# Gate logits with the weights held still in four 128x32 tiles, the partial products turned back and summed on VectorE

## The reference

```
attention:  per batch (8) and head (8): x 512x64, state 32x64
            xread = softmax(x state^T / 8) state,  sread = softmax(state x^T / 8) x
            rows = [xread, sread] per batch, heads side by side  -> 4608 tokens x 512
moe:        y = leaky_relu(rows @ w_in (512x2048), 0.01) @ w_out (2048x512)
moe2:       logits = y @ w_gate (512x8);  e = argmax(logits)
            gate = softmax(logits)[e],  eom = sigmoid(y @ w_output_gate (512x8))[e]
            out  = gate * eom * (relu(y @ w1[e]) @ w2[e])         8 experts, 1024 hidden
```

## Time and profile before

| what | value |
|---|---|
| time, median of 3 | 1213.87 us (1213.4 to 1214.17) |
| profiled execution, its own time | 1215.19 us |
| its span | 1212.8 us |
| PE busy | 1172.3 us, 97% |
| PEld (weight loads, beside PE) | 972.4 us, 80% |
| DVE busy | 564.4 us, 47% |
| ACT busy | 396.1 us, 33% |
| granted TensorE clock, mean | 0.994 of full |
| gate logits L531 on PE | 272 records, 32.7 us |

### The profile page before, as it was taken

One profiled execution on the slowest core, in us unless ns is written; L12 is line 12 of the kernel. 1 busy time (PEld: TensorE's weight loads), 2 busy tenths in 40 slices (PEclk: granted clock), 3 DMA queues, 4 the chain that ended last, 5 costly groups with the idle time before them and its releaser, 6 DMA issues.

```text
span 1212.8 us, 18414 instructions
## 1 busy us (share of the span) xinstructions
PE 1172.3 (97%) x6802; PEld 972.4 (80%) x6803; DVE 564.4 (47%) x1254; ACT 396.1 (33%) x743; POOL 160.0 (13%) x200
## 2 busy tenths in 40 slices
PE   5999999999999999999999997999999999999995
PEld 3778778778787777787787886898999989889894
DVE  5574373563654744744734436452222225355221
ACT  4343333333423433433333334141111124244111
POOL 1000001010010010010000104222112122233221
PEclk9999999999999999999999999899999999999998
DMA  9211111111120210110000320453111111533111
GB/s 354 98 40 35 36 40 36 35 40 36 40 70 1 73 37 6 69 36 1 35 1 1 112 81 35 122 203 114 35 52 36 51 53 43 191 99 118 51 37 34
DMA packets 37725, 78.44 MB, mean 65 GB/s; under 512 B 9094, under 2 KB 9350, under 8 KB 37639
## 3 DMA queue, kind: packets, MB, share of 16 engines
q1 hardware_dynamic: 28549, 52.92, 12.5%
q0 software_dynamic: 9120, 24.76, 6.5%
HBM read 59.75 MB, written 20.61 MB: 66 GB/s over the span
## 4 chain that ended last, share of the span: by engine, by line
PE 79%; DVE 13%; ACT 5%; issue 1%; DMA 0%; DVEq 0%; ACTq 0%; POOL 0%; SPq 0%; POOLq 0%
PE bank L462 22%; PE bank L464 22%; PE bank L463 22%; PE bank L531 2%; PE bank L513 2%; PE bank L562 2%; DVE gT_lo L1039 2%; PE bank L482 2%; ACT gT_hi L862 2%; DVE g_buf L1035 2%; PE bank L699 1%; PE bank L523 1%; DVE a_buf L1010 1%; DVE a_buf L1000 1%; ACT a2T L815 1%
## 5 line engine op out<-in xcount | busy, mean ns | idle before, releaser
L462 PE MATMUL bank<-wout_lo,gT_hi 128*128 128x512 f32 x544 | 219.1, 403 | 0.0
L464 PE MATMUL bank<-wout_hi,gT_hi 128*128 128x512 f32 x544 | 212.8, 391 | 0.0
L463 PE MATMUL bank<-wout_hi,gT_lo 128*128 128x512 f32 x544 | 211.9, 390 | 0.0
L462 PE MATMUL bank<-xgT_lo,w_hi 128*128 128x256 f32 x512 | 146.6, 286 | 2.7 <-DVE w_lo L1149 1.1
L464 PE MATMUL bank<-xgT_hi,w_hi 128*128 128x256 f32 x512 | 146.1, 285 | 0.0
L463 PE MATMUL bank<-xgT_hi,w_lo 128*128 128x256 f32 x512 | 146.1, 285 | 0.0
L1035 DVE TENSOR_TENSOR g_buf<-g_buf,bank 128x512 f32<-128x512 f32 (+1 forms) x144 | 94.4, 655 | 107.4 <-ACT g_buf L856 107.2
L856 ACT ACTIVATE g_buf<-bank 128x512 f32<-128x512 f32 (+1 forms) x144 | 82.8, 575 | 183.5 <-PE bank L464 157.7
L1039 DVE TENSOR_TENSOR gT_lo<-g_buf,gT_hi 128x512 fp32r<-128x512 f32 (+1 forms) x144 | 95.5, 663 | 91.4 <-ACT gT_hi L862 90.7
L933 ACT ACTIVATE hT_hi<-bank 128x256 fp32r<-128x256 f32 x128 | 48.9, 383 | 240.6 <-PE bank L464 240.6
L862 ACT CAST gT_hi<-g_buf 128x512 fp32r<-128x512 f32 (+1 forms) x144 | 85.9, 596 | 120.8 <-DVE g_buf L1035 120.8
(11 more groups left out here) (184 smaller groups left out, 1732.3 us busy)
## 6 DMA issues: line engine op xcount, KB each, us to landing
raw<-w_dram SPq DMA_DIRECT2D x20, 1024.0 KB, 8.0
rows_dram<-y_buf SPq DMA_DIRECT2D x8, 1032.0 KB, 4.6
XT<-xT_in_dram SPq DMA_DIRECT2D x8, 1024.0 KB, 5.3
X<-x_in_dram SPq DMA_DIRECT2D x8, 1024.0 KB, 5.1
win<-w_in_dram SPq DMA_DIRECT2D x4, 1024.0 KB, 13.5
y_buf<-w_out_dram POOLq DMA_DIRECT2D x6, 512.0 KB, 6.6
stT<-stT_in_dram SPq DMA_DIRECT2D x8, 128.0 KB, 2.2
yT<-w_out_dram POOLq DMA_DIRECT2D x2, 512.0 KB, 7.6
```

Source lines behind the costliest of these rows:

```text
L462: pe.matmul(o, l_hi, r_lo, start=first, stop=False)
L463: pe.matmul(o, l_lo, r_hi, start=False, stop=False)
L464: return pe.matmul(o, l_hi, r_hi, start=False, stop=last)
```

## The change

For routing r, each of the four turned tiles is kept until all are there. The turned rows of tiles 0 and 1 lie in `yT`, those of 2 and 3 in `scT` (free at that time; in layer 8 in a free part of the arena). `logit_parts` then holds a 128x32 piece of the gate weights still (16 real columns, 16 of no use) and lets 256 turned tokens stream by, in column group c for feature piece c: 4 groups, 2 halves of tokens, 8 fp32 multiplications. The four partial products lie under one another in one PSUM bank, 32 partitions each. ACT copies the bank (`keep_parts`), TensorE turns it back in four transposes (`flip_parts`), and DVE adds the four pieces while reading (`add_logits`). Flip 2 moves from f=4 to the end of f=3 and flip 3 from the end of f=4 to its middle. The logits of the state rows stay as they were (`state_logits`).

```diff
+        late_turned = at("late_turned", [P, 2, DM], fp32, offset=arena + 16 * 1024)
+        late_parts = at("late_parts", [P, DM], fp32, offset=arena + 20 * 1024)
+        def turned_pair(r, q):
+            return yT if q == 0 else scT if r < B - 1 else late_turned
+        def parts_of(r):
+            return a2T[:, 0, :] if r < B - 1 else late_parts
 flip_y:
-                    last = pe.transpose(aux[[0, 1, 1, 0][t]][:, P * c:P * c + P], y_buf[:, t, P * c:P * c + P], ident)
+                    last = pe.transpose(aux[t % 2][:, P * c:P * c + P], y_buf[:, t, P * c:P * c + P], ident)
-            def logits(r, q):
-                pe.wait_ge(yT_ready, 4 * r + 2 * q + 2)
-                for t in (0, 1):
-                    for c in range(DC):
-                        last = pe.matmul(aux[q][:, WG_N * t:WG_N * t + WG_N], yT[:, t, P * c:P * c + P], wg[:, WG * c:WG * c + WG_N],
-                                         start=(c == 0), stop=(c == DC - 1))
+            def logit_parts(r):
+                pe.wait_ge(gates_in, 16)
+                pe.wait_ge(yT_ready, 4 * r + 4)
+                for q in range(2):
+                    for c in range(DC):
+                        last = pe.matmul(aux[0][NS * c:NS * c + NS, PAIR * q:PAIR * q + PAIR], wg[:, WG * c:WG * c + NS],
+                                         turned_pair(r, q)[:, :, P * c:P * c + P], start=True, stop=True)
+                last.then_inc(parts_ps, 1)
+            def flip_parts(r):
+                pe.wait_ge(parts_kept, r + 1)
+                for t in range(4):
+                    last = pe.transpose(aux[1][:, P * t:P * t + P], parts_of(r)[:, P * t:P * t + P], ident)
+                last.then_inc(lg_ps, 1)
 beside_up, f == 4:
-                    flip_y(r, 2)
+                    else:
+                        pe.wait_ge(yT_ready, 4 * r + 2)
+                    flip_y(r, 3)
 beside_down:
   f == 3 
-                    logits(r, 0)
+                    else:
+                        pe.wait_ge(yT_ready, 4 * r + 1)
+                    flip_y(r, 2)
   f == 4 
-                    pe.wait_ge(lg_copied, 2 * r + 1)
-                    flip_y(r, 3)
+                    logit_parts(r)
   f == 5 
-                    logits(r, 1)
+                    flip_parts(r)
   f == 6, before make_v(b, 2)
-                        pe.wait_ge(lg_copied, 2 * r + 2)
+                        pe.wait_ge(lg_copied, r + 1)
 ScalarE
+            def keep_parts(r):
+                act.wait_ge(parts_ps, r + 1)
+                act.copy(parts_of(r)[:, :], aux[0][:, :]).then_inc(parts_kept, 1)
 beside_g:
                 if r is not None and f in (1, 2, 4):
-                    keep_yT(r, f // 2)
+                    keep_yT(r, f - 1)
+                elif r is not None and f == 5:
+                    keep_parts(r)
 layer, after g_step:
-                        if f == 4:
-                            keep_yT(r, 3)
+                        if f == 3:
+                            keep_yT(r, 2)
 VectorE, at f == 5 (before: at f == 3 and f == 5, copy_logits)
+            def add_logits(r):
+                dve.wait_ge(lg_ps, r + 1)
+                parts = aux[1][:, :].rearrange("p (t c e) -> p t e c", t=4, c=DC)
+                dve.reduce_sum(logit[:, :, :], parts[:, :, 0:WG, :], AX.X).then_inc(lg_copied, 1)
```

More of the change, by code:

```diff
@@ L188, in build @@
         yT_ps, yT_ready, lg_ps, lg_copied = sem("yT_ps"), sem("yT_ready"), sem("lg_ps"), sem("lg_copied")
+        parts_ps, parts_kept = sem("parts_ps"), sem("parts_kept")
         dif_ready, edif_ready, hot_ready, z_ready, ez_ready = sem("dif_ready"), sem("edif_ready"), sem("hot_ready"), sem("z_ready"), sem("ez_ready")
@@ L522, in flip_y, with state_logits @@
                 for c in range(DC):
-                    last = pe.transpose(aux[[0, 1, 1, 0][t]][:, P * c:P * c + P], y_buf[:, t, P * c:P * c + P], ident)
+                    last = pe.transpose(aux[t % 2][:, P * c:P * c + P], y_buf[:, t, P * c:P * c + P], ident)
                 last.then_inc(yT_ps, 1)
-            def logits(r, q):
+            def logit_parts(r):
                 pe.wait_ge(gates_in, 16)
-                pe.wait_ge(yT_ready, 4 * r + 2 * q + 2)
+                pe.wait_ge(yT_ready, 4 * r + 4)
[9 more added lines that the diff above has]
+                last.then_inc(lg_ps, 1)
+            def state_logits():
+                pe.wait_ge(gates_in, 16)
+                pe.wait_ge(yT_ready, 4 * B + 2)
                 for t in (0, 1):
                     for c in range(DC):
-                        last = pe.matmul(aux[q][:, WG_N * t:WG_N * t + WG_N], yT[:, t, P * c:P * c + P], wg[:, WG * c:WG * c + WG_N],
+                        last = pe.matmul(aux[0][:, WG_N * t:WG_N * t + WG_N], yT[:, t, P * c:P * c + P], wg[:, WG * c:WG * c + WG_N],
                                          start=(c == 0), stop=(c == DC - 1))
@@ L762, in first_step_and_last_routing @@
                 flip_y(B, 1)
-                logits(B, 0)
+                state_logits()
                 pe.wait_ge(xg_lo_done, 2)
@@ L768, in first_step_and_last_routing @@
                         ranks(B, 2, rank_bank=oacc[0])
-                        pe.wait_ge(lg_copied, 2 * B + 1)
+                        pe.wait_ge(lg_copied, B + 1)
                     if f >= 4:
@@ L834, in keep_yT @@
                 act.wait_ge(yT_ps, 4 * r + t + 1)
-                act.copy(yT[:, t % 2, :], aux[[0, 1, 1, 0][t]][:, :]).then_inc(yT_ready, 1)
+                act.copy(turned_pair(r, t // 2)[:, t % 2, :], aux[t % 2][:, :]).then_inc(yT_ready, 1)
+            def keep_parts(r):
+                act.wait_ge(parts_ps, r + 1)
+                act.copy(parts_of(r)[:, :], aux[0][:, :]).then_inc(parts_kept, 1)
             def exp_gates(r, tiles):
@@ L1046, in keep_y, with copy_state_logits @@
                     dve.tensor_copy(y_buf[:, t, 0:DM], acc[t][:, :]).then_inc(y_kept_v, 1)
-            def copy_logits(r, q):
-                dve.wait_ge(lg_ps, 2 * r + q + 1)
-                dve.tensor_copy(logit[:, 2 * q:2 * q + 2, :], aux[q][:, 0:2 * WG_N].rearrange("p (t n) -> p t n", t=2)[:, :, 0:WG]).then_inc(lg_copied, 1)
+            def add_logits(r):
+                dve.wait_ge(lg_ps, r + 1)
+                parts = aux[1][:, :].rearrange("p (t c e) -> p t e c", t=4, c=DC)
+                dve.reduce_sum(logit[:, :, :], parts[:, :, 0:WG, :], AX.X).then_inc(lg_copied, 1)
+            def copy_state_logits():
+                dve.wait_ge(lg_ps, B + 1)
+                dve.tensor_copy(logit[:, 0:2, :], aux[0][:, 0:2 * WG_N].rearrange("p (t n) -> p t n", t=2)[:, :, 0:WG]).then_inc(lg_copied, 1)
             RS = route_steps(4)
@@ L1060, in route @@
                 l1, l2 = logit[:, 0:T, 0:E], logit[:, 0:T, E:2 * E]
-                dve.wait_ge(lg_copied, 2 * r + T // 2)
+                dve.wait_ge(lg_copied, r + 1)
                 step = Steps(dve, route_step, RS * r, 6)
@@ L1159, in layer @@
                     if r is not None:
-                        if f in (3, 5):
-                            copy_logits(r, f // 2 - 1)
+                        if f == 5:
+                            add_logits(r)
                         elif f == 6:
@@ L1310, in _ @@
             rows_lo(0)
-            copy_logits(B, 0)
+            copy_state_logits()
             route(B, 2)
```

## The result

The changed kernel took 1199.53 us (median of 4, 1198.72 to 1200.67) against 1214.02 us for the kernel before: ratio 0.9878, 95% interval 0.9866 to 0.989, 14.5 us less. The forecast was 1199.1 us, with a range of 1197.2 to 1204.5. The profiled execution took 1198.8 us with a span of 1197.0 us, 15.8 us less than the span before.

A forecast was written before the change was run, and what follows sets the result against it. TensorE (PE) alone was taken to set a layer's length. Per routing 3.57 - 1.27 - 0.46 = 1.84 us less, 14.8 us over eight: 1215.2 - 14.8 = 1200.4 us, as a median 1199.1 us, range 1197.2 to 1204.5.

The forecast's parts named there:

- PE sets the length of a layer: Layers: PE busy 83.9 of 84.1 us, so PE work taken out shortens the kernel equally, unless a new wait opens.
- Removed, 3.57 us a routing: Old logits on PE: two calls per routing at 1.79 us each, 3.57 us together, go away.
- `logit_parts`, 1.27 us, four groups at once: New multiplications on PE: four column groups work at once, so a call costs 1.27 us; forecast's chance 0.76.
- The 0.05 us set aside for loads of a tile in use: In `logit_parts`: a tile's second multiplication loads weights only while its first runs; 0.05 us allowed.
- The lower end: Lower bound for a `logit_parts` call: 1.22 us, with nothing for loading the second multiplications' weights.
- Cover of `keep_parts`: ACT's new copy ends before `flip_parts` needs it: 1.3 us cover in layers 1 to 7, 0.17 in layer 8.
- DVE and transfers at nothing: DVE's sum takes 0.4 us, within 39 us of room per layer; no transfer added or moved; no cost.
- First rival, strict order: In `logit_parts`, a record with a busy tile holds back all behind: call 2.29 us, kernel 1207.3 us; chance 0.07.
- the 3.9 us: Length of `make_v` if multiplications start and end strictly in program order: about 9 x 0.43 us.
- Second rival, no concurrency: In `logit_parts`, tiles taking all 128 rows do not overlap: call 3.81 us, kernel 1219.5 us, slower; chance 0.05.
- From execution to median: Whole kernel: median of runs lies 1.3 us below the profiled execution, so 1200.4 us becomes 1199.1 us.

The follow-up runs named there:

- one-group run: Changed kernel with all eight `logit_parts` multiplications in column group 0, summed in PSUM, DVE reading only that piece: 1218.89 us, ratio 1.0037 to the kernel before.
- narrow-stream run: Kernel before, with 32 instead of 96 columns streaming in each multiplication of the old logits: 1213.98 us, ratio 0.9999.
- the run with the other order: Changed kernel with both token halves of a column group directly behind one another, then the next group: 1198.5 us, ratio 0.9871 to the kernel before.
- A second copy: Changed kernel with a second full ACT copy of the bank, into a buffer nobody reads, ahead of `keep_parts`: 1198.88 us, ratio 0.9877 to the kernel before.
- calls of 64: Changed kernel with `read_states` as thirty-two multiplications in one call, four column groups, and one transpose back: 1198.9 us, ratio 0.9858 to the kernel before.
- a kernel that differed in the place of the next waiting transpose: Kernel with `read_states` in two calls of sixteen multiplications (1187.71 us), its transpose moved behind `down(15)`, DVE keeping its result after the y copies: 1184.53 us.

## Why the prediction was right, step by step

- **PE sets the length of a layer.** Held. 3.58 us of old calls less 1.21 and 0.44 is 1.93 us, and the layer is 1.93 us shorter. In the one-group run a call longer by 2.56 us made the layer 2.52 us longer.
- **Removed, 3.57 us a routing.** Held, and the narrow-stream run shows that the columns were not what it paid for.
- **`logit_parts`, 1.27 us, four groups at once.** The mechanism held, as the one-group run shows; the size was 1.21. The 0.05 us set aside for loads of a tile in use was not needed. This and rounding in the flips (0.44, not 0.46) are the 0.09 us a routing by which the sum was short: 14.8 forecast, 8 x 1.93 = 15.4 in the layers.
- **The lower end.** The bound of 1.22 "with nothing for it" was in effect the value. The page "TensorE: Matmul & The Clock Gate" of the Trainium skill, section "Measured speedup vs the span model", gives 2.38 times for three column tiles, from which the prediction made an estimate of 1.09 us of streaming. The trace does not agree for the streaming: 1.21 less the 0.35 for the ends is 0.86 us.
- **Cover of `keep_parts`.** Held in layers 1 to 7. In layer 8 it held partly by luck. The prediction measured its cover against the start of the transposes, 1.58 us after `down`, but their weight loads need the copy and begin at 694.68, 1.34 us after `down` (693.34). A copy ending at 1.41 us, as worked out, would have come 0.07 us late. It ended at 1.24, because it began 0.27 us after the scaling and not 0.43, and 0.1 us of cover was left. A second copy used it up and cost 0.2 us once.
- **DVE and transfers at nothing.** Held: the sum takes 0.425 us where 0.4 was said, and in the stretch after layer 8 PE is busy for 7.41 of 14 us as before.
- **First rival, strict order.** Wrong, but the argument against it was weaker than the prediction put it. In `make_v` no tile is used by two multiplications, so all eight can start in the order of the program and still overlap; rows 5 then do not contradict the rule that the prediction quoted from the Trainium skill, and the 3.9 us that the prediction drew from it holds only if the rule is read for records and not for multiplications. The run with the other order is the proof.
- **Second rival, no concurrency.** Worked out at 1219.5 us; made on purpose it took 1218.9.
- **From execution to median.** The profiled executions differ by 16.4 us in time (15.8 in span), the medians by 14.5: the execution profiled before lay 1.2 us above its median, the one after 0.7 below. So the forecast's closeness (0.4 us) owes something to chance; the layers show an error of 0.6 us over all eight routings.

## What to carry to other kernels

Look for multiplications with few moving columns whose records follow each other 0.11 us apart under 128x128 weights. There cutting columns gives nothing, but holding the narrow operand still in four column groups turned 3.57 us into 1.21 plus 0.44 for turning back. Price it by the cost of entering and leaving (0.35 us a call) and by one group's streaming, and check the way back: a copy and a transpose need cover on their engines, and the cover ends where the weight load starts, not where the multiplication does. Calls of 16 and 32 narrow records ran without gaps here, calls of 64 in three cases of eight; nothing between was tried. A wait for the answer that stood 24 plain multiplications behind the call cost nothing, one that stood 12 behind cost 0.4 to 0.5 us in six layers.

## What the runs showed of the hardware that was not expected

- The four column groups of 128x32 tiles stream beside one another at no cost: 0.86 us for all four, 3.42 us for the same work in one.
- Multiplications for a free column group start ahead of an earlier one whose group is busy: the call costs 1.21 us in one order and 1.23 in the other.
- 64 records of narrow multiplications in a row stalled in five of eight calls, with gaps of 0.16 to 0.5 us (1.1 in two calls) after some 42 records. After two of the five the granted clock fell to 0.50 to 0.60 of full in stretches of 2 us, and plain multiplications stepped at 0.43 us for 3 to 3.5 us. Calls of 32 records did not stall.
- A signal came 3.0 us after the records that gave it had ended, DVE and the queue of the next X load both seeing it late (264.85 and 264.84), and came at once in a kernel that differed in the place of the next waiting transpose. Not explained.
